# Expert stage in three rounded terms, with the weights stationary and streamed, and the feed-forward for two experts at a time

## What is computed

```python
scores = scale * np.matmul(q, k.transpose(0, 1, 3, 2)) - np.log(S)     # 4 x 12 heads, S = 448, head_dim 64
attn = 1.0 / (1.0 + np.exp(-scores))
x = np.matmul(attn, v)                         # as rows: N = 1792 tokens, D = 768
logits = x @ w_gate                            # E = 8 experts, cap = N // E = 224
for idx in np.argsort(-logits.flatten()):      # greedy: best pair of token and expert first
    if assigned[tok] >= 0 or counts[e] >= cap: continue
    assigned[tok] = e
h = np.maximum(x[mask] @ w1[e], 0.0)           # w1: 768 x 1024 per expert
out[mask] = h @ w2[e]                          # w2: 1024 x 768 per expert
h = out @ w_in                                 # w_in: 768 x 2048, the same for all tokens
g = np.maximum(h, 0.0) + alpha * np.minimum(h, 0.0)
return g @ w_out                               # w_out: 2048 x 768
```

## Time and profile before

| | |
|---|---|
| median of the runs | 1190.31 us |
| the profiled execution, and its span from first to last instruction | 1192.4 us, 1190.8 us |
| TensorE matmul busy | 1088.2 us (91%) |
| VectorE busy | 704.0 us (59%) |
| ACT busy | 381.5 us (32%) |
| POOL busy | 154.5 us (13%) |
| DMA | 96.75 MB, 81 GB/s over the span |
| mean granted TensorE clock | 0.966 |

### The profile page before, as it was taken

One profiled execution on the slowest core, in us unless ns is written; L12 is line 12 of the kernel. 1 busy time (PEld: TensorE's weight loads), 2 busy tenths in 40 slices (PEclk: granted clock), 3 DMA queues, 4 the chain that ended last, 5 costly groups with the idle time before them and its releaser, 6 DMA issues.

```text
span 1190.8 us, 20756 instructions
## 1 busy us (share of the span) xinstructions
PE 1088.2 (91%) x6440; PEld 1004.3 (84%) x6440; DVE 704.0 (59%) x2988; ACT 381.5 (32%) x834; POOL 154.5 (13%) x182
## 2 busy tenths in 40 slices
PE   5999999107899999999999999999999999999996
PEld 3666665107899999999999999999999999999996
DVE  2333332785856865786578658766865786550352
ACT  3655555001124312521351134124311521351243
POOL 0000000013040004001300230031004001300000
PEclk9999999656999999999999999999999999999998
DMA  9859763015051006002400340042006002400000
GB/s 140 202 118 218 197 128 141 24 40 196 1 170 67 24 14 222 0 24 94 142 0 24 107 129 9 16 156 80 24 2 223 11 24 72 165 1 24 1 1 24
DMA packets 85352, 96.75 MB, mean 81 GB/s; under 512 B 69152, under 2 KB 69280, under 8 KB 85280
## 3 DMA queue, kind: packets, MB, share of 16 engines
q0 software_dynamic: 18688, 79.44, 20.1%
q1 hardware_dynamic: 65664, 16.52, 8.4%
q10 hardware_dynamic: 928, 0.03, 0.0%
HBM read 84.97 MB, written 11.01 MB: 81 GB/s over the span
## 4 chain that ended last, share of the span: by engine, by line
PE 81%; DVE 12%; issue 3%; another core or an unknown queue 2%; ACT 1%; DMA 1%; SPq 0%; DVEq 0%; POOL 0%; ACTq 0%; POOLq 0%
PE psum L541 42%; PE psum L581 21%; PE psum L447 6%; PE psum L432 6%; DVE hits L861 2%; PE psum L416 1%; PE psum L464 1%; PE psum L518 1%; DVE miss L879 1%; DVE spread L862 1%; DVE below L819 1%; DVE w_low L807 1%; DVE spread_own L863 1%; PE psum L457 1%
## 5 line engine op out<-in xcount | busy, mean ns | idle before, releaser
L541 PE MATMUL psum<-xT,w_in_sb 128*128 128x224 f32 x1536 | 299.6, 356 | 5.4 <-issue 5.4
L541 PEld LDWEIGHTS psum<-xT,w_in_sb 128*128 128x128 f32 x1536 | 290.8, 191 | 7.8 <-issue 7.2
L581 PE MATMUL psum<-w_high,g_high 128*112 128x384 f32 x512 | 176.1, 344 | 0.3 <-DVE w_low L807 0.3
L807 DVE TENSOR_TENSOR w_low<-w_out_sb,w_high 128x384 fp32r<-128x384 f32 x256 | 138.6, 556 | 61.6 <-ACT w_high L654 55.4
L581 PE MATMUL psum<-w_high,g_low 128*112 128x384 f32 x512 | 172.8, 338 | 0.0
L581 PE MATMUL psum<-w_low,g_high 128*112 128x384 f32 x512 | 172.5, 337 | 0.0
L654 ACT CAST w_high<-w_out_sb 128x384 fp32r<-128x384 f32 x256 | 131.7, 514 | 120.0 <-PE psum L581 120.0
L541 PE MATMUL psum<-xT,w_sb 128*128 128x224 f32 x768 | 148.9, 356 | 0.5 <-issue 0.5
L819 DVE SCALAR_TENSOR_TENSOR below<-below,neg_alpha,above 128x224 f32<-128x224 f32 x128 | 57.7, 451 | 153.4 <-ACT below L670 131.2
L541 PEld LDWEIGHTS psum<-xT,w_sb 128*128 128x128 f32 x768 | 146.9, 192 | 1.3 <-issue 0.9
L541 PE MATMUL psum<-hT,w_sb 128*128 128x224 f32 x768 | 146.6, 352 | 0.0
(11 more groups left out here) (114 smaller groups left out, 1042.0 us busy)
## 6 DMA issues: line engine op xcount, KB each, us to landing
w_in_sb<-in_moe_w_in_dram POOLq DMA_DIRECT2D x4, 1536.0 KB, 7.6
w_out_sb<-in_moe_w_out_dram POOLq DMA_DIRECT2D x4, 1536.0 KB, 11.6
q_in<-in_q_dram SPq DMA_DIRECT2D x24, 224.0 KB, 3.8
k_in<-in_k_dram SPq DMA_DIRECT2D x24, 224.0 KB, 5.7
v_in<-in_v_dram SPq DMA_DIRECT2D x24, 224.0 KB, 5.2
x_rows<-x_tok POOLq DMA_DIRECT2D x8, 672.0 KB, 5.7
w_sb<-in_moe_w_dram,w_idx POOLq DMA_INDIRECT x112
stage<-x_rows,tok_idx POOLq DMA_INDIRECT x16
```

The lines of the kernel that those rows point to most:

```text
L541: last = pe.matmul(psum[0:rows, s % TILE_BANKS, 0:cols], lhs(c), rhs(c), start=(c == 0), stop=(c == chunks - 1))
L581: last = pe.matmul(psum[0:P, s % TILE_BANKS, 0:HALF], g[:, c, t * P:(t + 1) * P], w[:, u % UNIT_RING, :], start=(c == 0 and i == 0), stop= ...
L807: dve.tensor_tensor(w_low[:, u % UNIT_RING, :], unit_of(w_out_sb, u), w_high[:, u % UNIT_RING, :].bitcast(F32), ALU.subtract).then_inc(w_s ...
```

## The change

All four products of an expert become three rounded terms each, and in all of them the weights are stationary (128x128 blocks) and the activations move: 224 columns for the expert's own w1 and w2 (`hidden`, `returned`), 448 columns, the tokens of two experts side by side, for w_in and w_out (`ffn_in`, `ffn_out`). The program now has four groups of two experts. In each group TensorE makes 60 steps, one for each unit of weights: 14 for the first expert (6 units of w1, 1024 columns wide, and 8 of w2, 768 wide), 14 for the second, then 32 for the feed-forward (16 of w_in and 16 of w_out in turn, 768 wide).

No weight stays in SBUF. Each unit comes by DMA into a ring `raw` of 16 (own ones gathered by POOL, those of the feed-forward loaded by SP), ACT rounds it into a ring `high` of 10, and VectorE subtracts to get `low`. So w_in and w_out are loaded, rounded and split once for each pair of experts. The activations are split too: the gathered tokens (`round_sel`, `split_sel`), h (`round_h`, `split_h`) and y (`round_y`, `split_y`). The rounding of g goes from VectorE to ACT (`round_g`). The result comes out with the features on the partitions, so that TensorE transposes it back (`turn_rows`) ahead of the scatter.

The routing is laid over the steps by numbers: `SUIT_AT`, `THR_AT`, `FLAGS_AT`, `IDX_AT` and `SEL_AT` name the step ahead of which TensorE does each small product of round r. In VectorE's program `go(s)` does all that is due up to step s, and `rank` calls it ahead of each bit with a target that runs evenly from SUIT_AT to THR_AT. The second expert's whole round comes ahead of step 14, and its `limit` keeps `go` at step 13 until `rank(1)` and `fill(1)` are through.

```diff
+    RAW_RING = 16
+    HIGH_RING = 10
+    LEAD = 6
...
+        def w1_unit(r, c):
+            return STEPS * (r // 2) + OWN * (r % 2) + c
...
+        def in_unit(q, m):
+            return STEPS * q + 2 * OWN + max(2 * m - 1, 0)
+
+        def out_unit(q, m):
+            return STEPS * q + 2 * OWN + min(2 * m + 2, 2 * FC - 1)
...
+        for r in range(1, E):
+            at = STEPS * (r // 2 - 1)
+            if r == 1:
+                SUIT_AT[r], THR_AT[r], FLAGS_AT[r], IDX_AT[r] = -1, OWN, OWN, OWN
+                SEL_AT[r] = [OWN] * PIECES
+            elif r % 2 == 0:
+                SUIT_AT[r], THR_AT[r], FLAGS_AT[r], IDX_AT[r] = at + (-2 if r > 2 else OWN + 1), at + 29, at + 31, at + 33
+                SEL_AT[r] = [at + 38 + i for i in range(PIECES)]
+            else:
+                SUIT_AT[r], THR_AT[r], FLAGS_AT[r], IDX_AT[r] = at + 35, at + 52, at + 54, at + 56
+                SEL_AT[r] = [at + STEPS + 5 + i for i in range(PIECES)]
...
+            def load(u, rows):
+                sp.wait_ge(unit_used, u - RAW_RING + 1)
+                to = raw[:, u % RAW_RING, 0:D]
+                if rows.shape[1] == DC:
+                    to = to.rearrange("p (c f) -> p c f", c=DC)
+                sp.dma_start(to, rows).then_inc(loaded(u)[0], 16)
+
+            for duo in range(GROUPS):
+                for m in range(FC):
+                    load(in_unit(duo, m), w_in_p[:, :, 128 * m:128 * m + 128])
+                    if m > 0:
+                        load(out_unit(duo, m - 1), w_out_p[:, m - 1, :])
+                load(out_unit(duo, FC - 1), w_out_p[:, FC - 1, :])
...
-            def expert(r, more, more2):
-                pe.wait_ge(sel_copied, SELS * (r + 1))
-                pe.wait_ge(w1_gathered, 16 * DC * (r + 1))
-                for m in range(EC):
-                    product(r, H0 + m, 128, CAP, lambda c: w1_sb[:, c, 128 * m:128 * m + 128],
-                            lambda c: xT[:, c, :], DC)
...
-                    product(r, G0 + m, 128, CAP, lambda c: w_in_sb[:, c, 128 * m:128 * m + 128],
-                            lambda c: yT[:, c, :], DC,
...
-                        for i, (g, w) in enumerate(((g_high, w_high), (g_high, w_low), (g_low, w_high))):
-                            last = pe.matmul(psum[0:P, s % TILE_BANKS, 0:HALF], g[:, c, t * P:(t + 1) * P],
...
+            def hidden(r):
+                for c in range(DC):
...
+                    pe.wait_ge(w_split, u + 1)
+                    for m in range(EC):
+                        to = psum[:, H_BANK + m // 2, CAP * (m % 2):CAP * (m % 2) + CAP]
+                        for i, (w, x) in enumerate(((high, x_high), (high, x_low), (low, x_high))):
+                            last = pe.matmul(to, part(w, u, m), x[r % 2][:, c, :],
...
                     last.then_inc(unit_used, 1)
...
+                    pe.wait_ge(h_split, EC // 2 * r + c // 2 + 1)
+                    pe.wait_ge(w_split, u + 1)
...
+                        for i, (w, h) in enumerate(((high, h_high), (high, h_low), (low, h_high))):
+                            last = pe.matmul(to, part(w, u, m), h[:, c, :],
...
+            def ffn_in(q, m):
+                u = in_unit(q, m)
+                routing(u)
+                if m > 0:
+                    pe.wait_ge(in_taken, FC * q + m)
+                pe.wait_ge(w_split, u + 1)
+                for c in range(DC):
+                    if m == 0:
+                        pe.wait_ge(y_split, DC // 2 * (2 * q + 1) + c // 2 + 1)
+                    for i, (w, y) in enumerate(((high, y_high), (high, y_low), (low, y_high))):
+                        last = pe.matmul(psum[:, IN_BANK, 0:PAIR], part(w, u, c), y[:, c, :],
+                                         start=(c == 0 and i == 0), stop=(c == DC - 1 and i == 2))
+                last.then_inc(unit_used, 1)
+
+            def ffn_out(q, m):
+                u = out_unit(q, m)
+                routing(u)
+                pe.wait_ge(g_split, FC * q + m + 1)
...
+                for d in range(DC):
+                    for i, (w, g) in enumerate(((high, g_high), (high, g_low), (low, g_high))):
+                        last = pe.matmul(psum[:, OUT_BANK + d, 0:PAIR], part(w, u, d), g[:, m % 2, :],
...
+                last.then_inc(unit_used, 1)
...
+            for piece in range(PIECES):
+                turn_sel(0, piece)
+            for q in range(GROUPS):
+                for r in (2 * q, 2 * q + 1):
+                    hidden(r)
+                    returned(r)
+                for m in range(FC):
+                    ffn_in(q, m)
+                    if m > 0:
+                        ffn_out(q, m - 1)
+                ffn_out(q, FC - 1)
...
+            def round_units(upto):
+                while rounded[0] < min(upto, LAST):
+                    u = rounded[0]
+                    act.wait_ge(*loaded(u))
+                    if u >= HIGH_RING:
+                        act.wait_ge(unit_used, u - HIGH_RING + 1)
+                    act.copy(high[:, u % HIGH_RING, 0:width(u)], raw[:, u % RAW_RING, 0:width(u)]).then_inc(w_rounded, 1)
+                    rounded[0] += 1
...
+            def take_in(q, m):
+                act.wait_ge(unit_used, in_unit(q, m) + 1)
+                act.activation(above[:, m % 2, :], psum[:, IN_BANK, 0:PAIR], ACT.Relu)
+                act.activation(below[:, m % 2, :], psum[:, IN_BANK, 0:PAIR], ACT.Relu, scale=-1.0).then_inc(in_taken, 1)
+
+            def round_g(q, m):
+                act.wait_ge(g_made, FC * q + m + 1)
+                act.copy(g_high[:, m % 2, :], below[:, m % 2, :]).then_inc(g_rounded, 1)
...
-            def split_w(r, u):
-
-                dve.wait_ge(w_rounded, unit(r, u))
-                dve.tensor_tensor(w_low[:, u % UNIT_RING, :], unit_of(w_out_sb, u),
-                                  w_high[:, u % UNIT_RING, :].bitcast(F32), ALU.subtract).then_inc(w_split, 1)
...
+            def split_units(upto):
+                while split[0] < min(upto, LAST):
+                    u = split[0]
+                    dve.wait_ge(w_rounded, u + 1)
+                    dve.tensor_tensor(low[:, u % RAW_RING, 0:width(u)], raw[:, u % RAW_RING, 0:width(u)],
+                                      high[:, u % HIGH_RING, 0:width(u)].bitcast(F32), ALU.subtract).then_inc(w_split, 1)
+                    split[0] += 1
...
+            def prelu(q, m):
+                g = below[:, m % 2, :]
+                dve.wait_ge(in_taken, FC * q + m + 1)
+                dve.scalar_tensor_tensor(out=g, in0=g, scalar=neg_alpha[:, m:m + 1], in1=above[:, m % 2, :],
+                                         op0=ALU.mult, op1=ALU.add).then_inc(g_made, 1)
+
+            def split_g(q, m):
+                dve.wait_ge(g_rounded, FC * q + m + 1)
+                dve.tensor_tensor(g_low[:, m % 2, :], below[:, m % 2, :], g_high[:, m % 2, :].bitcast(F32),
+                                  ALU.subtract).then_inc(g_split, 1)
...
+            def go(s):
+
+                while gone[0] <= min(s, limit[0], LAST - 1):
+                    s0 = gone[0]
+                    q, k = s0 // STEPS, s0 % STEPS
+                    for i in range(2):
+                        if k == OWN * i + DC:
+                            split_h(2 * q + i)
+                        if k == OWN * i + OWN:
+                            split_y(2 * q + i)
+                    for r in range(1, E):
+                        for piece in range(PIECES):
+                            if s0 == SEL_AT[r][piece]:
+                                split_sel(r, piece)
+                    for m in range(FC):
+                        if s0 == in_unit(q, m) + 2:
+                            split_g(q, m)
+                    for m in range(FC):
+                        if s0 == in_unit(q, m) + 1:
+                            prelu(q, m)
+                    split_units(OWN if s0 < OWN and s0 + LEAD >= OWN else s0 + LEAD + 1)
+                    gone[0] += 1
...
                 for bit in range(BITS - 1, -1, -1):
-                    split_some()
+                    if r == 1 and bit == BITS - 3:
+                        for piece in range(PIECES):
+                            split_sel(0, piece)
+                        split_units(LEAD)
+                    if r > 1 or (r == 1 and bit <= BITS - 3):
+                        go(SUIT_AT[r] + (THR_AT[r] - SUIT_AT[r]) * (BITS - bit) // (BITS + 1))
```

More of the change, by code:

```diff
@@ L296, in tile @@
[L296 to L306, removed]
+        OWN = DC + EC
+        STEPS = 2 * OWN + 2 * FC
+        LAST = GROUPS * STEPS
+        def w1_unit(r, c):
+            return STEPS * (r // 2) + OWN * (r % 2) + c
@@ L405, in _ @@
+            for r in range(2):
+                gather_w1(r)
+                gather_x(r)
+                gather_w2(r)
+            for q in range(GROUPS):
+                for r in range(2 * q + 2, min(2 * q + 4, E)):
+                    gather_x(r)
+                    gather_w1(r)
+                    gather_w2(r)
+                scatter(q)
```

(29 more changed lines are left out.)

508 lines of the change are left out of this document (275 added, 233 removed).

## The result

The changed kernel takes 1218.5 us (median of 4 runs, 1217.1 to 1223.1) against 1190.6: a ratio of 1.024, 95% interval 1.021 to 1.027. It is **slower by 2.4%**, where faster was forecast. The median lies in the range of 1140 to 1240, but 44 us above the 1174 that was predicted. The profiled execution has a span of 1216.2 us.

The account below looks back on a forecast made before the run. TensorE bounds the expert stage now; changed, it (191 us a group) ties with VectorE (189.5). Sum: 441 + 24 + 69 + 24 = 558, two more periods 964, last group 1160, tail to span 1174.5: 1174 us, range 1140 to 1240.

Parts of the forecast that it names:

- Prices of TensorE: TensorE's rounded products: 0.111 us for 224 columns, 0.204 for 448; 191 us a group of two experts against 222.
- the rival that reads load records as the array's time: Weight loads set the pace: 224-column products cost 0.19 us, 45.5 us more a group, 1304 us; chance 0.09.
- The start: Up to step 29, a chain on VectorE: thresholds at 343.2 and 439.5, step 29 at 441; costs 90 us.
- Odd ranks: Odd round's rank, steps 35 to 52: TensorE 64 us, VectorE 68.6, taken as 69.
- Its fill, steps 29 to 35: TensorE 22 + 1.8 = 24: Fill after an even round's rank: TensorE 24 us, VectorE 18.
- I take 86: Even round's rank, from two steps before the group to step 29: 83 us on each engine, taken as 86 with meetings.
- The fills behind odd ranks: Odd round's fill, from step 52 to step 58: 24 us.
- meeting at each h and y: Even rank: TensorE and VectorE, 83 us each, meet at each h and y, so 86 us is taken.
- VectorE waits inside its ranks: Rival: each unit's split waits for ACT, 0.47 us at 127 units, 60 us more, 1234 us; chance 0.20.
- The balance: Whole kernel: TensorE's cheaper products alone would give 125 us, of which the start costs 90; 1174 us forecast.
- ACT and DMA: Covered beside TensorE and VectorE: ACT some 100 of 203 us a group, loads at most 76 us.

Follow-up runs that it names:

- 16 bits: Rank searches only the 16 highest bits where there were 31: on the kernel before 1164.4 us, on the changed kernel 1122.1 us.
- the interleaved start: Changed kernel with rounds 1 and 2 splitting each token piece ahead of one bit, round 2's rank begun before the second expert's tokens: 1204.2 us.
- narrower splits: Changed kernel with VectorE splitting only 128 of 768 columns of a feed-forward unit from unit 44 on, TensorE's work the same: 1195.7 us.
- the shorter fills: Changed kernel with other table numbers: each fill takes four steps instead of six, ranks of rounds 3 to 7 get two more: 1196.3 us.
- the paced run: Changed kernel with the step due at each bit in rounds 3 to 7 following the time of TensorE's steps, not their number: 1210.0 us.

## Why the prediction was wrong

- *Prices of TensorE*: right. 0.111 was chosen between 0.102 and 0.19, the rows show 0.11; 0.204 shows 0.203. The record of a 128x128 load is still 0.19 us while products follow every 0.11, so the rival that reads load records as the array's time is out. The Trainium skill's "Perfetto Trace Analysis", § Identifying the Most-Contended Engine, gives the busy share of the weight loads, beside MFU, as the measure of how near TensorE is to its limit. Here the trace does not agree for that share: it stood at 97% in the expert stage before (107.9 of 111.1 us), and yet about as many loads (6536 for 6440) now go with 78 us less of TensorE's time.
- *The start*: right in every step. First own product at 290.4 (about 289 was forecast), `rank(1)` at 342.8 (343.2), the first of expert 1's tokens at 362.8 (362.8), round 2's threshold at 438.2 (439.5). The two experiments that touch it (16 bits, the interleaved start) confirm a chain on VectorE.
- *Odd ranks*: right, 69.6 for 69, and on VectorE, since both lighter ranks and narrower splits bring them to 63.
- **The step that failed** is the listing of a group's pieces: "Its fill, steps 29 to 35: TensorE 22 + 1.8 = 24" and "I take 86" for the even rank. The first took TensorE to be busy through steps in which the feed-forward's pipeline has just begun: w_in's first product, the copies, PReLU, rounding and split must be through before the first product of w_out, and I had not followed ACT's order there (`take_in(1)` ahead of `round_g(0)`). These fills took 29.9, 28.3 and 29.9 us instead of 24, which is 16 us, and the last group's start has the same waits, in the 5 us of the table's last row. The run with that order turned gave back 18 of these 21. The low clock after waits was not in the sum either, about 1.5 us each time; I had put it under VectorE's chain and looked for it at the start alone. The fills behind odd ranks, right but for this, lost their 7 us for the most part by it.
- In the even rank the failed term is the 3 us for "meeting at each h and y" on top of 83 against 83. TensorE waited 10.7 and 9.3 us there, and the stretches took 94.5 and 91.9. A stretch was priced by each engine's total in it, but the chain of work runs over TensorE in its first part and over VectorE in the rest, and what VectorE loses by waiting in the first it can't regain in the second. The chain and the waits in the trace show this, and the shorter fills and the paced run gave part of it back. How the 14 us divide between that, the low clock and the late start into the stretch was not separated. Nor was an order tried in which ACT rounds the next unit ahead of its copies of the last group's rows.
- *The rival "VectorE waits inside its ranks"* had the right side and a nearby time (1234). Its mechanism, VectorE waiting for ACT and ACT standing in its own order behind a product, is there, but in the first steps of the even ranks alone: five waits of 1.1 to 3.1 us each time. Its price, 0.47 us at each unit of each rank, is not: the odd ranks had no such waits. That its time lies near is mostly luck.
- *The balance*: the 16 us of gain that were forecast are what is left of much larger terms, 125 gained and 90 lost at the start alone. An error of 42 us in the span turned the sign.
- ACT and DMA stayed covered: 39% busy, and some 38% of the sixteen engines' time by the page's queues; 134.8 MB instead of 96.8 cost TensorE no visible wait but the two for the tokens at the start (7.7 us the longest), and the first of these stands in the kernel before too.

## What to carry to other kernels

When a change lifts the load of a second engine to that of the first, add the stretches one by one, each at the slower engine, and then the starts and ends of each pipeline inside a period: half of the error here lay in a few steps that happen once a group. Two engines in a fixed order with equal totals can take longer than either total, when one is slower in the first part of a stretch and the other in the rest; so compare them part by part. Numbers in a table, which name the step at which one may go on, were worth 22 us. And ask where an operation stands in its own engine's queue behind another that waits for a later product.

## What the runs showed of the hardware

A rounded product of 128x128 weights and 224 columns started every 0.11 us though its weight load has a record of 0.19 to 0.20 us. After idle times of only 2.9 to 3.2 us TensorE's clock fell to half for some 3.4 us in eight cases of twelve, and it stayed at full in the four others, one of them behind the same 2.91 us at the same place of a group. After 1.0 to 1.6 us it did not fall. In the run with shorter fills it fell behind two idle times of 2.0 and 2.1 us and stayed at full behind another of 2.0.
